# Seven half-size products for eight in the dense up product of an attention and two-layer expert kernel, with its weight splits and sums on GpSimd

## The reference

```python
kv = einsum('bhsd,bhse->bhde', k, v)            # 4 batches, 8 heads, 576 rows, 64 wide
o = einsum('bhsd,bhde->bhse', q, kv)
x = o / sqrt(mean(o * o) + 1e-6) * g_norm       # as rows: x is 2304 tokens x 512
p = domain_probs / (sum(domain_probs) + 1e-9)   # 4 dense experts
for e in range(4):                              # w1: 512 x 1024, w2: 1024 x 512
    x1 += p[:, e:e + 1] * (maximum(x @ w1[e], 0) @ w2[e])
# then 8 routed experts: one expert per token by cosine with expert_emb, times its gate
out[mask] = gate[mask] * (maximum(x1[mask] @ w1b[e], 0) @ w2b[e])
```

## Time and profile before

| | |
|---|---|
| device time, 3 runs | 1214.83, 1215.43, 1217.95 us (median 1215.43) |
| the profiled execution | span 1213.2 us from its first to its last instruction; what a device time holds around a span is some 2 us |
| attention stage | to 80.0 us, where the first `up` begins |
| dense stage | 80.0 to 903.6 us, the last `add` |
| routing's end, tables, scatter | to 921.7 us |
| routed stage | to 1213.2 us |

### The profile page before, as it was taken

One profiled execution on the slowest core, in us unless ns is written; L12 is line 12 of the kernel. 1 busy time (PEld: TensorE's weight loads), 2 busy tenths in 40 slices (PEclk: granted clock), 3 DMA queues, 4 the chain that ended last, 5 costly groups with the idle time before them and its releaser, 6 DMA issues.

```text
span 1213.2 us, 19048 instructions
## 1 busy us (share of the span) xinstructions
PE 1182.5 (97%) x6472; PEld 1051.9 (87%) x6473; DVE 557.4 (46%) x873; ACT 327.5 (27%) x493; POOL 66.3 (5%) x84
## 2 busy tenths in 40 slices
PE   8989999999999999999999999999988999999996
PEld 8879999999999999999999999999977888888884
DVE  5875455455454554455455554453563121212211
ACT  5752212122222212222112122122771122222211
POOL 3010000000000000000000000000131111111100
PEclk9999999999999999999999999999998999999999
DMA  9904343523525325343353443552697958518960
GB/s 236 254 19 171 139 167 128 191 109 133 190 104 190 137 105 195 127 162 140 125 189 117 156 156 121 193 197 105 227 331 275 365 192 323 195 51 316 379 226 13
DMA packets 88298, 216.75 MB, mean 179 GB/s; under 512 B 27973, under 2 KB 42309, under 8 KB 80080
## 3 DMA queue, kind: packets, MB, share of 16 engines
q1 hardware_dynamic: 83296, 201.66, 47.0%
q0 software_dynamic: 4800, 14.72, 3.3%
q10 hardware_dynamic: 176, 0.02, 0.0%
HBM read 137.44 MB, written 79.98 MB: 179 GB/s over the span
## 4 chain that ended last, share of the span: by engine, by line
PE 91%; ACT 2%; DVE 2%; issue 1%; DMA 1%; SPq 1%; POOL 0%; DVEq 0%; ACTq 0%; POOLq 0%
PE ps L1001 29%; PE ps L1003 29%; PE ps L1002 29%; PE ps L1156 2%; ACT xT_parts L473 1%; DVE xT_parts L637 1%; PE ps L1077 1%; PE ps L1122 1%; DMA kvq<-in_q_dram 1%; PE ps L940 1%; PE ps L951 1%; PE ps L1064 1%; SPq L226 0%; PE ps L962 0%; SPq L223 0%
## 5 line engine op out<-in xcount | busy, mean ns | idle before, releaser
L1001 PE MATMUL ps<-xT_parts,w_hi 128*128 128x384 f32 x768 | 258.8, 337 | 0.0
L1003 PE MATMUL ps<-xT_parts,w_lo 128*128 128x384 f32 x768 | 258.5, 337 | 0.0
L1002 PE MATMUL ps<-xT_parts,w_hi 128*128 128x384 f32 x768 | 257.8, 336 | 0.0
L722 DVE SCALAR_TENSOR_TENSOR x_rows<-ps,dense_prob_col,x_rows 128x512 f32<-128x512 f32 x288 | 215.2, 748 | 85.5 <-PE ps L1003 85.5
L521 ACT ACTIVATE hT_hi<-ps 128x768 fp32r<-128x768 f32 x96 | 78.1, 814 | 586.3 <-PE ps L1003 586.3
L709 DVE SCALAR_TENSOR_TENSOR hT_lo<-ps,hT_hi 128x768 fp32r<-128x768 f32 x96 | 91.9, 957 | 292.8 <-ACT hT_hi L521 292.8
L1003 PE MATMUL ps<-w_hi,hT_lo 128*128 128x512 f32 x576 | 226.1, 392 | 0.0
L1002 PE MATMUL ps<-w_lo,hT_hi 128*128 128x512 f32 x576 | 225.9, 392 | 0.0
L1001 PE MATMUL ps<-w_hi,hT_hi 128*128 128x512 f32 x576 | 225.2, 391 | 0.1
L1001 PEld LDWEIGHTS ps<-xT_parts,w_hi 128*128 128x128 f32 x768 | 144.8, 188 | 3.5
L1002 PEld LDWEIGHTS ps<-xT_parts,w_hi 128*128 128x128 f32 x768 | 144.7, 188 | 3.5
(11 more groups left out here) (159 smaller groups left out, 1072.0 us busy)
## 6 DMA issues: line engine op xcount, KB each, us to landing
w_slots<-split_parts SPq DMA_DIRECT2D x64, 1024.0 KB
ahead_raw<-in_moe_w_dram SPq DMA_DIRECT2D x64, 512.0 KB, 3.4
split_parts<-ahead_hi SPq DMA_DIRECT2D x64, 512.0 KB, 2.7
split_parts<-ahead_lo SPq DMA_DIRECT2D x64, 512.0 KB, 3.4
w_raw<-in_moe_w_dram SPq DMA_DIRECT2D x32, 512.0 KB, 5.3
row_tile<-dispatched_rows POOLq DMA_DIRECT2D x20, 257.0 KB, 6.0
kvq<-in_k_dram SPq DMA_DIRECT2D x16, 288.0 KB, 5.1
kvq<-in_v_dram SPq DMA_DIRECT2D x16, 288.0 KB, 6.2
```

The source lines that it names most:

```text
L722: V.scalar_tensor_tensor(acc[:, t, 0:D], ps[:, bank, :], pcol[:, uu, t:t + 1], acc[:, t, 0:D], ALU.mult, ALU.add).then_inc(y_used, 1)
L1001: mm(out_, ah, bh, start=(first and m == 0), stop=False)
L1002: mm(out_, ah, bl, start=False, stop=False)
L1003: last = mm(out_, al, bh, start=False, stop=(final and m == n - 1))
```

## The change

**Products.** The dense `up` now takes 768 tokens, a third, at once. Tokens are halved (384 and 384), the 512 rows of w1 are halved (256 and 256) and its 256 columns too (128 and 128), and the product of these 2 by 2 blocks is made by Winograd's form of Strassen's algorithm: seven products of half-size blocks, each with 2 chunks of the inner dimension and 3 matmuls, 42 matmuls of 384 columns for 768 tokens. Before, 768 tokens took 48.

**Order.** The thirds are outermost: for each third all 16 pieces of weights, so 48 steps of one `up` (42 matmuls) and one `down` (6 tiles, 36 matmuls, that of the step before). Each piece's weights are thus loaded and split three times.

**Operands.** Seven operands of x for each third, three of them sums made by POOL (`x_sums`) and one a difference written over x; high parts by ACT (`x_high`), low parts by POOL in the first third and by DVE (five) and POOL (two) in the others. Seven operands of w1 in each step: four sums by POOL (`w1_sums`), high parts by ACT (`w1_highs`), low parts by POOL (`w1_lows`). w2's low part is POOL's too (`w2_lows`). There is one raw buffer each for w1 and w2.

**Combination.** DVE adds the products out of PSUM (`combine`: u2, u3, c22, c21, c12), partly in SBUF, and makes four low parts of the hidden values; ACT copies the first product and makes four high parts. `add` is as before, six to a step.

**Ahead work.** Two chunks to a step in 32 of the 48 steps (`AHEAD_AT`: steps 1 to 14, 22 to 30, 38 to 46). The low part is now written over the raw chunk.

**Routing.** The first two thirds are routed within steps 18 to 23 and 34 to 39, the last behind the last step. The first routed weights are read back when all `up` are done. The attention loops are unrolled; `low_x` is gone from them, and ACT makes the first third's `x_high` in their last four units.

The core of the diff (names of buffers, the routing's banks and unchanged computation left out):

```diff
-    BT = 384
-    NB = NTOK // BT
-    BTT = BT // P
-    G = 2 * NB
+    THIRDS = 3
+    TK = NTOK // THIRDS
+    HT = TK // 2
+    TPT = TK // P
+    STEPS = THIRDS * NU
+    OPS = 7
...
+    AHEAD_AT = list(range(1, 15)) + list(range(22, 31)) + list(range(38, 47))
+    assert 2 * len(AHEAD_AT) == NAHEAD
...
+        def x_operand(t, i):
+            return (x_part(t, 0, 0), x_sum(t, 1), x_sum(t, 0), x_part(t, 1, 0), x_part(t, 0, 1), x_part(t, 1, 1), x_sum(t, 2))[i]
+        W_OF = (0, 4, 3, 5, 1, 6, 2)
...
-                    for c in range(CPU_):
-                        s = c % 2
-                        off = uu * 2 * WCOL + c // 2 * 2 * PIECE + c % 2 * CH
-                        w = sp.wait_ge(s_lo, (2 * i + uu) * CPU_ + c + 1)
-                        if not last:
-                            w.then_inc(sp_turns, 1)
-                        sp.dma_start(parts[i, :, off:off + CH], shi[:, s, :].bitcast(F32)).then_inc(s_out[s], 16)
-                        sp.dma_start(parts[i, :, off + PIECE:off + PIECE + CH], slo[:, s, :].bitcast(F32)).then_inc(s_out[s], 16)
...
-                        w = sp.wait_ge(s_out[s], 32 * ((2 * i + uu) * (CPU_ // 2) + c // 2 + 1))
-                        if not last:
-                            w.then_inc(sp_turns, 1)
-                        if c < CPU_ - 2:
-                            load_ahead(i, uu, c + 2, s)
...
+            for k in range(STEPS):
+                if k + 2 < STEPS:
+                    sp.wait_ge(w1_split, k + 2)
+                    load_w1(k + 2)
+                if k + 1 < STEPS:
+                    sp.wait_ge(w2_split, k + 1)
+                    load_w2(k + 1)
+                if k in AHEAD_AT:
+                    c = 2 * AHEAD_AT.index(k)
+                    store_ahead(c)
+                    store_ahead(c + 1)
+                    for s in range(2):
+                        if c + 2 + s < NAHEAD:
+                            sp.wait_ge(s_out[s], 32 * (c // 2 + 1))
+                            load_ahead(c + 2 + s)
...
+            def w1_sums(k):
+                pool.wait_ge(w1_in, 16 * (k + 1))
+                if k:
+                    pool.wait_ge(w1_hi, 3 * k)
+                    pool.wait_ge(w1_split, k)
+                g.tensor_tensor(tsum[:, 0], w1_block(0, 1), w1_block(0, 0), ALU.subtract).then_inc(w1_summed, 1)
+                g.tensor_tensor(tsum[:, 2], w1_block(1, 1), w1_block(0, 1), ALU.subtract).then_inc(w1_summed, 1)
+                pool.wait_ge(w1_summed, 4 * k + 1)
+                g.tensor_tensor(tsum[:, 1], w1_block(1, 1), tsum[:, 0], ALU.subtract).then_inc(w1_summed, 1)
+                pool.wait_ge(w1_summed, 4 * k + 3)
+                g.tensor_tensor(tsum[:, 3], w1_block(1, 0), tsum[:, 1], ALU.subtract).then_inc(w1_summed, 1)
+            def w1_lows(k):
+                s = k % 2
+                pool.wait_ge(w1_hi, 3 * k + 2)
+                g.tensor_tensor(w1l[s][:, 0:2], w1_raw4[:, :, :, 0:P], w1h[s][:, 0:2].bitcast(F32), ALU.subtract)
+                g.tensor_tensor(w1l[s][:, 2], w1_block(1, 1), w1h[s][:, 2].bitcast(F32), ALU.subtract)
+                pool.wait_ge(w1_hi, 3 * k + 3)
+                pool.wait_ge(w1_summed, 4 * k + 4)
+                g.tensor_tensor(w1l[s][:, 3:7].rearrange("p m c n -> p (m c n)"), tsum[:, :, :, :].rearrange("p m c n -> p (m c n)"),
+                                w1h[s][:, 3:7].rearrange("p m c n -> p (m c n)").bitcast(F32), ALU.subtract).then_inc(w1_split, 1)
+            def w2_lows(k):
+                s = k % 2
+                pool.wait_ge(w2_hi, k + 1)
+                g.tensor_tensor(w2l[s][:, :, :].rearrange("p c n -> p (c n)"), w2raw[:, :, :].rearrange("p c n -> p (c n)"),
+                                w2h[s][:, :, :].rearrange("p c n -> p (c n)").bitcast(F32), ALU.subtract).then_inc(w2_split, 1)
...
+                if k + 1 < STEPS:
+                    w1_lows(k + 1)
+                if k + 2 < STEPS:
+                    w1_sums(k + 2)
+                w2_lows(k)
+                if t + 1 < THIRDS and 8 <= k % NU < 12:
+                    x_sums(t + 1, k % NU - 8)
...
+            def combine(k):
+                s = k % 2
+                if k:
+                    dve.wait_ge(h_hi, 4 * k)
+                    dve.wait_ge(h_lo, 4 * k)
+                dve.wait_ge(p1_copied, k + 1)
+                dve.wait_ge(up_done, OPS * k + 2)
+                V.tensor_tensor(u2[:, :], ps[:, 1, 0:HT], p1[:, :], ALU.add).then_inc(u2_done, 1)
+                dve.wait_ge(up_done, OPS * k + 4)
+                V.tensor_tensor(u3[:, :], ps[:, 1, 0:HT], p1[:, :], ALU.add).then_inc(u3_done, 1)
+                dve.wait_ge(u3_done, k + 1)
+                V.tensor_tensor(c22[:, :], ps[:, 2, 0:HT], u3[:, :], ALU.add).then_inc(c22_done, 1)
+                dve.wait_ge(h_hi, 4 * k + 1)
+                V.scalar_tensor_tensor(hl[s][:, 0, 0:HT], ps[:, 0, 0:HT], 0.0, hh[s][:, 0, 0:HT].bitcast(F32), ALU.max, ALU.subtract).then_inc(h_lo, 1)
+                dve.wait_ge(up_done, OPS * k + 6)
+                dve.wait_ge(c22_done, k + 1)
+                V.tensor_tensor(u3[:, :], ps[:, 3, 0:HT], u3[:, :], ALU.add).then_inc(c21_done, 1)
+                dve.wait_ge(h_hi, 4 * k + 2)
+                V.scalar_tensor_tensor(hl[s][:, 1, HT:TK], c22[:, :], 0.0, hh[s][:, 1, HT:TK].bitcast(F32), ALU.max, ALU.subtract).then_inc(h_lo, 1)
+                dve.wait_ge(up_done, OPS * k + 7)
+                dve.wait_ge(u2_done, k + 1)
+                V.tensor_tensor(u2[:, :], ps[:, 2, 0:HT], u2[:, :], ALU.add).then_inc(c12_done, 1)
+                dve.wait_ge(h_hi, 4 * k + 3)
+                V.scalar_tensor_tensor(hl[s][:, 0, HT:TK], u3[:, :], 0.0, hh[s][:, 0, HT:TK].bitcast(F32), ALU.max, ALU.subtract).then_inc(h_lo, 1)
+                dve.wait_ge(h_hi, 4 * k + 4)
+                V.scalar_tensor_tensor(hl[s][:, 1, 0:HT], u2[:, :], 0.0, hh[s][:, 1, 0:HT].bitcast(F32), ALU.max, ALU.subtract).then_inc(h_lo, 1)
...
-            def up(b, s, us):
-                gr = slice(b * (BT // SUB), (b + 1) * (BT // SUB))
-                for f in range(FC):
-                    fs = slice(f * P, (f + 1) * P)
-                    last = three(ps[:, 2 * s + f, 0:BT].rearrange("p (g n) -> p g n", n=SUB),
-                                 [(w1h[us][:, c, fs], w1l[us][:, c, fs], xp[:, gr, 0, c, :], xp[:, gr, 1, c, :]) for c in range(KC)])
-                last.then_inc(h_done, 1)
...
+            def product(k, i, bank, first=True, final=True):
+                s, m = k % 2, W_OF[i]
+                if k % NU == 0:
+                    x_ready(k, i)
+                three(ps[:, bank, 0:HT], [(w1h[s][:, m, c, :], w1l[s][:, m, c, :], xoh[:, i, c, :], xol[:, i, c, :]) for c in range(2)],
+                      first, final).then_inc(up_done, 1)
+            def up(k, flipped, chosen, ranked):
+                pe.wait_ge(w1_split, k + 1)
+                if flipped:
+                    pe.wait_ge(xt_copied, flipped)
+                if k:
+                    pe.wait_ge(h_lo, 4 * (k - 1) + 1)
+                product(k, 0, 0, True, False)
+                if k:
+                    pe.wait_ge(u3_done, k)
+                product(k, 1, 1, True, False)
+                if k:
+                    pe.wait_ge(c12_done, k)
+                if chosen:
+                    pe.wait_ge(lg_read, chosen)
+                product(k, 2, 2, True, False)
+                pe.wait_ge(u2_done, k + 1)
+                product(k, 3, 1, False, True)
+                pe.wait_ge(p1_copied, k + 1)
+                product(k, 4, 0, False, True)
+                if k == 0:
+                    transposed(UNITS - 1, 1)
+                if k:
+                    pe.wait_ge(c21_done, k)
+                if ranked:
+                    pe.wait_ge(rank_read, ranked)
+                product(k, 5, 3)
+                pe.wait_ge(c22_done, k + 1)
+                product(k, 6, 2, False, True)
+            def down(k, j):
+                s, n = k % 2, y_index(k, j)
+                if j == 0:
+                    pe.wait_ge(h_lo, 4 * (k + 1))
+                    pe.wait_ge(w2_split, k + 1)
```

More of the change, by code:

```diff
@@ L756, in _ @@
+            dve.wait_ge(consts_made, 14)
             steps = [0]
@@ L1051, in _ @@
-            with pe.Fori(0, TURNS - 1) as i:
-                for b in range(G):
-                    block(i, b)
-            for b in range(NB):
-                block(TURNS - 1, b)
-            def flip(t):
-                pe.wait_ge(y_used, (NU - 1) * TT + 4 + t + 1)
-                if t:
-                    pe.wait_ge(xt_copied, t)
+                    mm(out_, ah, bh, start=(first and m == 0), stop=False, skip_group_check=not final or not first)
+                    mm(out_, ah, bl, start=False, stop=False, skip_group_check=not final or not first)
@@ L1116, in flip_rows @@
+            T0 = TT - TPT
+            for n, (kk, j) in enumerate(TAIL):
+                down(kk, j)
+                if kk == LAST and j >= 1:
+                    flip(T0 + j - 1, LAST)
```

(7 more changed lines are left out.)

691 lines of the change are left out of this document (370 added, 321 removed).

## The result

| | before | changed |
|---|---|---|
| device time, four runs each | 1215.67 us (1214.83 to 1217.95) | 1407.82 us (1399.02 to 1417.55) |
| ratio | | 1.158, 95% interval 1.153 to 1.164 |
| span of the profiled execution | 1213.2 | 1416.0 |
| first up matmul to last slots | 80.01 to 910.7 | 83.63 to 1109.33 |

A forecast was written before the change was run, and what follows sets the result against it. PE's matmuls bound the old kernel; a loop of waits through SP, DMA and POOL would bind the new. -50.3 + 112 + 4.5 + 7 + 9 + 4 = +86 on 1213.2 gives span 1299.5, median 1302 us; range 1235 to 1365.

The forecast's parts named there:

- Part 1: Dense up matmuls on PE: 288 fewer, -50.3 us; a new step takes PE 15.57 us.
- Part 2: ACT and DVE in each dense step: some 7.5 and 12.3 us of work, both fitting in 15.57 us.
- Part 3: POOL in each dense step: 0.69 us per 256 elements, 9.6 us a step, which by itself fits.
- Part 4: Waits looping through SP, DMA and POOL in 32 ahead-work steps: 19.1 us against 15.57 of PE work, +112 us.
- The upper end, 20.7: Highest price of one turn of the loop through SP, DMA and POOL: 20.7 us, +164 us.
- Part 5: Start of the dense stage +4.5 us, first two steps +7, two changes of third +9, routing beside steps 0.
- Changes of third: At the two changes of third PE waits for w1 and w2 behind POOL's x lows: +9 us (0 to 20).
- Part 6: End of dense stage: last add to last slots 11 us instead of 7.1, +4 us (2 to 8).
- A: Rival: the loop of waits stays under 15.6 us and hides; -26, 1189 us, chance 0.10.
- B: Rival: a short loop of waits at its low end, 17.0 us a turn; 1236 us, chance 0.14.
- C: Rival: POOL and DVE exclude each other at SBUF, +1.2 us a loop; +42, 1344 us, chance 0.28.
- D: Rival: PE's clock drops after idle gaps, at most 1.7 us a step, fitting in the wait; no chance given.

The follow-up runs named there:

- exchange 1: Changed kernel with POOL making w2's low part ahead of the four w1 sums instead of behind them; 1288.1 us.
- both exchanges: Changed kernel with w2's low part ahead of the sums on POOL and w2's high part ahead of the ahead high parts on ACT; 1200.2 us, ratio 0.987.
- w1's load first: Changed kernel with SP issuing the next w1 load before the wait for stores and the two ahead loads; 1307.1 us.
- loads by ACT: Changed kernel with w1's and w2's loads issued from ACT's queue instead of SP's, POOL's order unchanged; 1222.2 us.
- the 1410.5: Changed kernel with three of DVE's low parts of the hidden values reading a PSUM bank instead of sums in SBUF; 1410.5 us.
- the fastest kernel: Kernel with both exchanges, plus w1's first high parts four units earlier on ACT and first low parts before POOL's x lows; 1187.9 us, ratio 0.977.

## Why the prediction was right or wrong

**Part 1, right.** 6184 matmuls, and a step where nothing waits is 15.5 us (15.57).

**Part 2, right in size.** DVE's 384 elements from PSUM took 0.55 to 0.56 (0.6), ACT's 0.47 to 0.53 (0.46). DVE's low parts from SBUF took twice that on average, in turns with POOL, and it did not matter to the step.

**Part 3, right.** POOL's 256 elements took 0.73 where nothing held them off (0.69), 1024 took 2.38 (2.37). The kernel without ahead work shows that POOL's load fits. The estimate of 0.78 from the Trainium skill (GPSIMD Engine Reference, 3.1 Elementwise) was as near, on the other side.

**Part 4, the step that failed.** The mechanism and its place stood as written: the order of waits on SP, not the amount of anything. Four experiments that changed only an order or the queue of the loads (exchange 1, both exchanges, w1's load first, loads by ACT) bring 101 to 208 us, and the one that took three of DVE's five turns away nothing. What failed is the price of the loop: 22.2 us a turn for 19.1 in the first third. Over the twelve turns that begin from 155.16 to 399.17, in the sum's own terms:

| piece | forecast | measured, mean |
|---|---|---|
| w1's load to the first sum | 4.9 | 5.9 |
| four sums | 2.8 | 3.8 |
| w2's low part | 2.4 | 2.4 |
| w2's load to the last ahead load | 8.1 | 9.8 |
| last ahead load to the w1 load | 0.9 | 0.4 |

The first piece was taken from a load behind one ahead load, and here there are two: it took mostly 3.4 to 3.9 us in the steps that had no ahead load before it, and mostly 4.7 to 7.3 in those that had. The sums are longer because the first or the second meets DVE's ahead low part (1.75 us on POOL at 294.38, beside one of 1.22 on DVE from 294.32); four take 2.8 to 2.9 where none does. The fourth piece I priced from the bytes' rate in a full stretch. In windows of 0.5 us the transfers start slowly:

```profile
301.50:302.00 0.50, 0.50 (x5) 0.50 (x4) 0.50 (x2) 0.20 (x1) 0.50 (x1) 1.00 0.45 74
302.00:302.50 0.50, 0.50 (x4) 0.46 (x3) 0.50 (x1) 0.33 (x1) 0.50 (x2) 1.00 0.65 98
...
303.50:304.00 0.50, 0.50 (x4) 0.41 (x3) 0.50 (x1) 0.42 (x1) 0.50 (x1) 1.00 1.24 442
```

The pair of the earlier trace rows had 106 GB/s in its first half microsecond too, so that the eight idle microseconds are the reason is not shown. The end was late as well: the last store, issued at 303.37, landed 7.7 us later, and SP went on at 311.08. Its issues do not explain the rest. The third and fourth store took SP 1.2 to 1.4 us each, but it was through with them at 304.74 and waited from there. How much of the 1.7 us is the start and how much the end is open. The upper end, 20.7, was short too: it took each piece at its largest single row, and none of those rows was taken in the contention that the change makes.

Over all 32 steps the excess above PE's work is 684.2 - 32 x 15.57 = 186 us for 112 forecast: of the 113 us by which the dense stage was longer than forecast, some 74 come from here.

**Part 5.** Start +3.6 (+4.5): right, though profiles with the same start differ by up to 5 us in it. First two steps 14.3 and 17.5 us for 7.3 and 15.6, +8.9 (+7): right; the second is among the 32 above as well. **Changes of third, wrong:** the four steps around them took 94.8 us against 62.3 of PE's work, +32.5 where +9 (0 to 20) was written. PE stood 11.2 us there at a time, until POOL had made w2's low part of the third's last step. That part stood behind the four sums, and these behind a w1 load that SP issued only at 422.01, behind the stores and two ahead loads:

```profile
428.70 0.72 POOL L445 TENSOR_TENSOR w_sums<-w_raw 128x256 f32<-128x256 f32 x1 [13.06 <-DMA w_raw<-in_moe_w_dram]
431.54 2.34 POOL L467 TENSOR_TENSOR w_lo<-w_raw,w_hi 128x1024 fp32r<-128x1024 f32 x1
433.98 0.77 PE L1136 MATMUL ps<-w_hi,hT_hi 128*128 128x512 f32 x1 [11.17 <-issue]
```

I had said that w2's low part is late there and taken it as paid in the 32 steps. It is paid on top, because `down` of that step precedes the new third. With both exchanges the same four steps take 63.8. **Routing beside the steps, at 0, was a little short:** in the kernel with both exchanges the four steps 18 to 21 take 73.8 us, 11.5 over PE's 62.3, for six tiles routed; before, six tiles lengthened two blocks from 8.31 to 12.46, 8.3 in all. For twelve tiles that is some 6 us more.

**Part 6, right.** Last add's end to last slots 9.8 us (7.1 + 4), +2.7 of a range of 2 to 8.

The rest of the 113, some 15 us, lies in the ten steps 17 to 21 and 33 to 37 (184.0 us) and in the end, from the copy of the last step's first product to the last slots (46.1). PE's own products are 155.7 and 22.8 of these, so 51.6 stand above them, where the forecast had 36.8 (830.7 - 797.9 of the kernel before, and part 6's 4). With both exchanges the two take 181.8 and 39.9, that is 43.2: some 8 of the 15 us go with the loop, and some 6 are the routing's.

**The rivals.** A named what would happen if the loop came under PE's step, 1189 us: built that way, by order alone, the kernel takes 1200.2, and 1187.9 with the start changed too. The terms outside part 4 were nearly right in sum, in part by luck: the changes of third cost 1.5 us there for the 9 forecast, and routing and the end 6 more than forecast. What made it slow was not the algorithm. B's short loop did not occur. C's mechanism is shown, and its price came in part. The sums on the loop did grow by 1.0 us a turn, nearly the 1.2 it had, from DVE's ahead low parts; that DVE's other instructions in turns cost time while the loop is long is refuted by the 1410.5. C's 1344 was the nearest of my figures, but most of the miss is not C's: no kernel took the ahead low parts alone out of the long loop. D: the granted clock was 0.91 on average over 89 to 1060 against 1.00 before, and busy matmul time 812.1 us for 3799 of them, against 745.5 for 3804 in the fastest kernel (100 to 860, granted 1.00). That is 67 us more, 2.1 in each of 32 steps, where I had written at most 1.7. So half clock was granted oftener than I thought. That it costs nothing because it lies in the wait, as I wrote, is argued and not shown: no run separates the clock from the waits.

## What to carry to other kernels

When a change adds a wait to an in-order queue, write out the ring that it closes (which issue waits for which result, back to itself), and look in it first for two neighbours that do not need each other: two exchanges of neighbours were worth 208 us here, and loads moved to another queue 186, with no operation removed. A ring's pieces are to be priced under the bursts that the ring makes: a load that lands behind others, transfers from their slow start to the landing of the last one, instructions beside those they take turns with. And lateness at a change of stage is paid a second time.
